# First tile of a fused attention and MLP kernel: splitting the weights of blocks 4 to 8 one block sooner

## The reference, cut to what matters

```python
q, k, v: [4, 8, 576, 64]                     # batch, heads, tokens, head size
# attention on means of 4 tokens, repeated 4 times, plus attention in a band of 7 tokens
x = (out_up + out_local)                     # -> [2304, 512]
y = (x @ w_a) * (x @ w_b) @ w_out            # w_a, w_b [512, 1536], w_out [1536, 512]
h = y @ w_in                                 # [512, 1024]
solu = h * softmax(h)
out = layernorm(solu) * g_ln @ w_out2        # [1024, 512]
```

## Time and profile before

| | |
|---|---|
| time, median of 3 executions | 777.87 us (775.64 to 778.09) |
| the profiled execution | 774.99 us, its span 773.2 us |
| TensorE busy | 758.6 us, 98% of the span |
| VectorE, ScalarE, GpSimd busy | 72%, 39%, 25% |
| TensorE's granted clock | 1.000 (2.4 GHz) |

### The profile page before, as it was taken

The page is one execution under the profiler, slowest core; times in us unless marked ns, Lnnn a source line. Parts: engine busy times, 40 slices in busy tenths (PEclk is TensorE's granted clock), DMA queues, the critical chain, the costliest instruction groups (busy, mean ns, idle before and its releaser), DMA issues.

```text
span 773.2 us, 12657 instructions
## 1 busy us (share of the span) xinstructions
PE 758.6 (98%) x4626; PEld 702.1 (91%) x4626; DVE 553.2 (72%) x980; ACT 300.8 (39%) x824; POOL 193.4 (25%) x236
## 2 busy tenths in 40 slices
PE   8999999999999999999999999999999999999998
PEld 7889888999999999999999999999988888888886
DVE  5799978879878887797877874023477666666663
ACT  4745546463524434362525343234422222222222
POOL 3348884275444030060001221111100000000000
PEclk9999999999999999999999999999999999999999
DMA  9999966768899575473746623726011111011011
GB/s 180 208 200 233 214 148 202 224 190 243 222 212 258 141 204 167 152 188 104 192 140 180 164 88 105 233 92 209 31 65 55 35 47 55 28 55 55 28 42 41
DMA packets 94651, 108.84 MB, mean 141 GB/s; under 512 B 29310, under 2 KB 62590, under 8 KB 94590
## 3 DMA queue, kind: packets, MB, share of 16 engines
q1 hardware_dynamic: 83293, 99.38, 49.4%
q10 hardware_dynamic: 11296, 8.65, 3.7%
HBM read 87.46 MB, written 20.55 MB: 140 GB/s over the span
## 4 chain that ended last, share of the span: by engine, by line
PE 90%; DVE 4%; SPq 2%; ACT 2%; issue 1%; DMA 1%; ACTq 0%; DVEq 0%
PE psum L950 27%; PE psum L952 26%; PE psum L951 26%; PE psum L1077 2%; PE psum L907 2%; PE psum L859 1%; PE psum L883 1%; PE psum L918 1%; DMA v_h<-in_v 1%; PE psum L893 1%; DVE tmp L1623 1%; DVE tmp L1575 1%; PE psum L732 1%; SPq L477 1%; SPq L471 1%
## 5 line engine op out<-in xcount | busy, mean ns | idle before, releaser
L950 PE MATMUL psum<-x_hi,w_hi 128*128 128x384 f32 x576 | 198.2, 344 | 2.3 <-DVE ab_f L1541 1.1
L952 PE MATMUL psum<-x_hi,w_lo 128*128 128x384 f32 x576 | 193.0, 335 | 0.0
L951 PE MATMUL psum<-x_lo,w_hi 128*128 128x384 f32 x576 | 192.8, 335 | 0.0
L950 PEld LDWEIGHTS psum<-x_hi,w_hi 128*128 128x128 f32 x576 | 108.2, 188 | 6.1 <-issue 4.4
L951 PEld LDWEIGHTS psum<-x_lo,w_hi 128*128 128x128 f32 x576 | 108.3, 188 | 0.0
L952 PEld LDWEIGHTS psum<-x_hi,w_lo 128*128 128x128 f32 x576 | 108.1, 188 | 0.0
L950 PE MATMUL psum<-ab_hi,wo_hi 128*128 128x384 f32 x288 | 99.5, 346 | 0.4 <-issue 0.4
L952 PE MATMUL psum<-ab_hi,wo_lo 128*128 128x384 f32 x288 | 96.5, 335 | 0.0
L951 PE MATMUL psum<-ab_lo,wo_hi 128*128 128x384 f32 x288 | 96.4, 335 | 0.0
L1541 DVE TENSOR_TENSOR ab_f<-psum,a_sb 128x384 f32<-128x384 f32 x72 | 39.9, 554 | 74.3 <-PE psum L952 53.9
L1260 ACT ACTIVATE a_sb<-psum 128x384 f32<-128x384 f32 x72 | 35.2, 488 | 107.6 <-PE psum L952 107.6
(11 more groups left out here) (163 smaller groups left out, 1429.7 us busy)
## 6 DMA issues: line engine op xcount, KB each, us to landing
wo_hi<-wo_hi_scratch SPq DMA_DIRECT2D x53, 256.0 KB, 2.7
wo_lo<-wo_lo_scratch SPq DMA_DIRECT2D x53, 256.0 KB, 3.2
wo_raw<-in_moe_w_out SPq DMA_DIRECT2D x19, 256.0 KB, 5.4
yT_scratch<-y_sb ACTq DMA_DIRECT2D x6, 768.0 KB, 6.2
y_raw<-yT_scratch SPq DMA_DIRECT2D x18, 256.0 KB, 3.0
out<-out_sb SPq DMA_DIRECT2D x18, 256.0 KB, 2.1
k_u<-in_k SPq DMA_DIRECT2D x11, 384.0 KB
v_u<-in_v SPq DMA_DIRECT2D x11, 384.0 KB
```

The costliest lines, as they stand in the source:

```text
L950: mm(dst, wh, xh, start=first, stop=False, skip_group_check=not check)
L951: mm(dst, wh, xl, start=False, stop=False, skip_group_check=not check)
L952: last = mm(dst, wl, xh, start=False, stop=end, skip_group_check=not check)
```

## The change

Three things change, all in the first tile. Blocks 4 to 8 are split one step sooner on ScalarE and GpSimd (blocks 4, 5, 6, 7, 8 in steps 1 to 5; before in steps 2, 3, 4, 5, 5). GpSimd's `pool_sums(1, 2, 1)` goes ahead of `wo_low(4)` and block 6. On ScalarE block 3 goes ahead of `ab_high(1)`, block 10 behind `a_copy(7)`, and block 11 from step 7 to the end of step 6. TensorE's, VectorE's and SyncE's lists stay as they are.

```diff
-SPLIT_AT = {0: (2,), 2: (4,), 3: (5,), 4: (6,), 5: (7, 8), 6: (9, 10), 7: (11,)}
+SPLIT_AT = {0: (2,), 1: (4,), 2: (5,), 3: (6,), 4: (7,), 5: (8,), 6: (9, 10, 11)}
 # ScalarE, in step j
                     if m == 0:
-                        for i in SPLIT_AT.get(j, ()):
+                        for i in SPLIT_AT.get(j, ())[:1]:
                             weight_high(i)
                     if g + 1 < FC * TILES:
                         a_copy(g + 1)
+                    if m == 0:
+                        for i in SPLIT_AT.get(j, ())[1:2]:
+                            weight_high(i)
                     from_tensor(m, 3 * j + 1)
                     of_units(m, 3 * j + 1)
                     from_tensor(m, 3 * j + 2)
+                    if g == 0:
+                        weight_high(HEAD_BLOCKS + 1)
...
                     of_units(m, 3 * j + 2)
-                    if g == 0:
-                        weight_high(HEAD_BLOCKS + 1)
+                    if m == 0:
+                        for i in SPLIT_AT.get(j, ())[2:]:
+                            weight_high(i)
 # GpSimd, in step j
-                    splits = SPLIT_AT.get(j, ()) if m == 0 and j > 1 else ()
+                    splits = SPLIT_AT.get(j, ()) if m == 0 and j > 0 else ()
+
+                    if m == 0 and j == 3:
+                        pool_sums(1, 2, 1)
+                        wo_low(g + 1)
                     for i in splits[:1]:
                         weight_low(i)
-                    if g > 0 and g + 1 < FC * TILES and wo_fresh(g + 1):
+                    if g > 0 and g + 1 < FC * TILES and wo_fresh(g + 1) and (m > 0 or j != 3):
                         wo_low(g + 1)
-                    if m == 0 and j == 3:
-                        pool_sums(1, 2, 1)
```

## The result

The changed kernel is slower: 783.67 us (median of 22 executions, 772.98 to 786.34) against 776.93 us of the kernel before beside it (22 executions, 773.06 to 779.89). The ratio is 1.0067, 95% interval [1.0047, 1.0086]. It leaves out executions more than 1.5% above the fastest, and since those of the changed kernel fall in two groups, four at 773.0 to 775.7 (mean granted clock 0.995 to 0.998) and eighteen at 782.7 to 786.3 (0.989 to 0.993), the medians say more: +6.7 us. The forecast was +1.5 us with a range up to 782.2. The median, 783.67, lies above it; by the ratio, 0.67% of 776.93 is 5.2 us and the time 782.1, just inside. Either way the change costs more than three times what the sum said.

What follows compares the result with a forecast made beforehand. TensorE's list was taken as the bound (758.6 of 773.2 us busy), so only its holes could change. 3.92 - 0.92 - 1.0 - 0.5 = +1.5 us on the median 777.87 gave 779.4 us, range 775.9 to 782.2.

Steps and rivals of the forecast that it cites:

- The wait for block 4: ScalarE in step 1 stands until block 4's weights land at 59.2, moving TensorE's slot 5 from 57.25 to 61.17: +3.92 us.
- Block 3: Ahead of ab_hi(1) on ScalarE: closes TensorE's 0.60 us hole at 54.35, worth nothing because TensorE then waits until 61.17.
- block 5's hole: TensorE's wait at 75.13 for GpSimd's split of block 5 goes, as the split comes earlier: -0.92 us.
- block 11: Leaving its place at 111.98 on ScalarE closes the hole at 113.95; -0.5 us taken for blocks 7 to 11, bounds 0 and 1.60.
- The holes at 78.58 and 81.34: TensorE's waits where VectorE is late (ab_f, down product): -1.0 us taken, from a range of 0 to 1.52 won back.
- The clock rival: TensorE's clock falls behind a 4.4 us hole at slot 5, costing 1.3 to 2.7 us: +3.1, or 781.0; chance 0.20.
- The stall is not given back: Rival: VectorE's long sum or wo_lo(4) is as late as TensorE after slot 5: +3.0, or 780.9 us; chance 0.20.

Runs made afterwards that it cites:

- e12: Kernel before, with block 4's split alone moved to step 1 on ScalarE and GpSimd: median 782.98 us, ratio 1.0097.
- e1: The changed kernel run again with no edit: median 783.60 us, ratio 1.0062 against the kernel before.
- e5: Changed kernel, with GpSimd waiting ahead of block 6's split until VectorE has made ab_lo(4): median 777.12 us, ratio 1.0012.
- e7: Changed kernel, with GpSimd's step 3 back in the old order (block 6's split, wo_low(4), sums): median 779.66 us, ratio 1.0052.
- e9: Changed kernel, with GpSimd waiting for ab_lo(4) behind block 6's split and ahead of block 7's: median 778.13 us, ratio 1.0034.
- e8: Kernel before, with only ScalarE's moves of blocks 3, 10 and 11 (block 8 also falls behind a_copy(6)): median 775.07 us, ratio 1.0000.
- e2: Changed kernel, with block 4's split back in step 2: median 777.58 us, ratio 1.0027.
- e4: Changed kernel, with block 4's high part still in step 1 but behind a_copy(2) and job 0's out_d on ScalarE: median 784.21 us, ratio 1.0125.
- e6: Kernel before, with block 6's split moved from step 4 to 3 and block 7's from 5 to 4: median 775.59 us, ratio 0.9987.
- e10: Changed kernel, with GpSimd's wait for ab_lo(4) ahead of block 6 and 30 filler products on TensorE at slot 5: median 776.40 us, ratio 1.0008.
- e3: Changed kernel, with 30 filler products on TensorE at slot 5 ahead of the wait for out_d: median 783.54 us, ratio 1.0075.
- e11: Changed kernel, with block 4 back in step 2, wo_low(4) ahead of the sums, and GpSimd waiting for ab_lo(4): median 776.70 us, ratio 1.0012.

## Why the prediction was right or wrong

**The wait for block 4.** Right in place and size. Landing at 59.2 and TensorE's slot 5 at 61.17 were forecast; e12 has 59.01 and 61.00, e1 59.75 and 61.73, e5 61.51. What the forecast took as given is that TensorE comes to slot 5 near 57: where half clock from 22 to 26 has made tile 0 late, the hole is 0.19 (after), 1.36 (e7) and 1.99 (e9).

**Block 3, block 5's hole, block 11.** Right: the holes at 54.35, 75.13 and 113.95 are gone in the profile after. Block 11's -0.5 is fair in that execution, where 0.55 + 0.41 + 0.64 became 1.12, but with ScalarE's moves alone (e8) it was nothing: the chain of VectorE behind it took all back, the bound I had named.

**The holes at 78.58 and 81.34: the step that failed.** The prediction took -1.0 us, with 0 and -1.52 as its ends. I had the row that mattered, one sum of 5.64 us beside block 5's split, and read it as a stretch that would be there again or not. The runs showed it to be a wait for a turn at the shared port, 8.2 to 9.6 us long in five profiles (e1, e2, e4, e6, e10) in which the pause near 82 is gone, and a hole on TensorE of 5.8 to 9.0 us when ab_lo(4) is the one to wait or is behind it. Where that happens the term has the wrong sign; e5 takes 6.5 us off the median by a pause of 0.5. That it happens in the executions of the upper group is seen in the two that were profiled, e1 and e4. I costed GpSimd's new order by the sum of its work (21.5 us) and asked when each result would be ready. I did not ask where its pauses went.
I cited the Trainium skill there ("SBUF — State Buffer", section "SBUF: two separate sides"): an exclusive lock, held for a whole instruction. The lock is what the traces show. One instruction as its length is not: VectorE waited through twelve of them in e1.

**The clock rival.** Right as a mechanism, and priced too low: behind holes of 5.1 and 5.8 us the granted clock is 0.50 over 6.5 us and 0.77 over 8.4 (e1), and with filler at slot 5 it stays at 1.00 (e3, e10). Its price at slot 5 was put at 1.3 to 2.7 us; the rows give some 3.2, and the second hole, which no term had, adds 1.9. e4 shows that the hole at slot 5 with its clock is not needed to make the kernel slow. This is also what the Trainium skill says ("TensorE: Matmul & The Clock Gate", section "HAM oscillation — how this bites in real kernels") of holes of this size, and the traces agree.

**The stall is not given back.** This rival had the right side and the wrong size, +3.0 us, as it too took a long sum of 5.6 us for the worst. That the ratio's 782.1 falls just inside the range owes nothing to the sum: its +1.5 has neither the second hole nor the clock. Slower by over 0.3% was given 0.36, within 0.3% 0.56. The profiled execution of before was one of its faster ones (774.99, median 776.9), and its clock of 1.00 is not that of all: others show 0.993 to 0.998.

## What to carry to other kernels

When two engines share a port, a pause in the one's list is a sure turn for the other, and without one the turn can come very late. Before work is moved forward to fill such a pause, look at what the other engine has to deliver then, and if TensorE waits for it, put a wait there: half a microsecond on the engine with slack bought 6.5. And a single instruction that takes ten times its usual length is a wait, not noise: find what it waits for, and ask what TensorE needs from behind it. A hole costs more than its length: count the half clock behind it too. Profile more than one execution when times stand in two groups; the one at hand may be of the wrong one.

## What the runs showed of the hardware

VectorE can be shut out over a long run of GpSimd's instructions: 9.04 us (e1), 9.46 (e2), 9.56 (e4), 8.22 (e6), 8.37 (e10), each over a run of GpSimd at full pace, 0.69 us for a split. In e1 and e10 it ended when GpSimd's list paused, in the other three between two instructions of GpSimd. In other executions of the same program the two take turns, 1.3 us for a split and 1.5 for a VectorE sum of 0.94. Which of the two comes is not set by the program alone: e3 had four executions of the one group and five of the other. What decides it is open. Within the rows read here, instructions of VectorE with one operand in PSUM (ab_f, 0.54 to 0.56 us) and its sums over rows (0.94) kept their length in the midst of it.

Behind holes of TensorE of about the same size the granted clock was low for very different times: 0.50 over 6.5 us behind 5.13 (e1), 0.57 over 19.1 us behind 4.37 (e11). What sets that length is open too.
